# The second layer's router logits: product-and-sum on VectorE in place of transposes and matmuls on TensorE

## The reference, cut to what matters

```python
out[mask] = gate_w[mask, None] * (h @ w2[e])    # first layer: its output rows, y here
...
logits = x @ w_gate                             # second layer: x = y, (3072, 512) @ (512, 8)
flat = logits.flatten()
order = np.argsort(-flat)                       # greedy assignment by this order
```

## Time and profile before

| | |
|---|---|
| median of 3 runs | 1130.14 us (1125.43 to 1133.53) |
| the profiled execution's own time | 1124.73 us |
| its span | 1123.0 us |
| first layer's tiles | about 250 to 619 us of the span |
| TensorE busy, whole span | 933.2 us (83%) |
| VectorE busy, whole span | 592.6 us (53%) |
| mean granted clock of TensorE | 0.92 |

### The profile page before, as it was taken

How to read it: one execution, slowest core, us unless ns; L and a number is a source line. 1 busy time by engine, 2 the same in 40 slices (tenths; PEclk the granted TensorE clock), 3 DMA queues, 4 the chain that set the end, 5 groups by cost and what they waited for, 6 DMA issues and landing times.

```text
span 1123.0 us, 22070 instructions
## 1 busy us (share of the span) xinstructions
PE 933.2 (83%) x7642; PEld 767.9 (68%) x7643; DVE 592.6 (53%) x1728; ACT 320.9 (29%) x651; POOL 207.1 (18%) x291
## 2 busy tenths in 40 slices
PE   5998989617999999999997226797978889798995
PEld 4786878515888888888886215676666767576884
DVE  5767566575222222222221587777776777776550
ACT  3455454324222222222221021131313122224230
POOL 6644333001111111111110001020202020202021
PEclk9999999758999999999998556898999989899998
DMA  9668684604011111111110041414131221407110
GB/s 198 132 123 170 128 161 94 177 18 170 29 38 38 39 41 43 38 38 38 38 38 20 14 151 29 150 58 151 58 148 56 103 99 68 141 18 286 73 48 29
DMA packets 46015, 97.86 MB, mean 87 GB/s; under 512 B 7248, under 2 KB 19584, under 8 KB 45952
## 3 DMA queue, kind: packets, MB, share of 16 engines
q1 hardware_dynamic: 27200, 59.55, 18.4%
q0 software_dynamic: 8064, 26.46, 7.5%
q10 hardware_dynamic: 10688, 11.01, 4.8%
HBM read 77.49 MB, written 19.51 MB: 86 GB/s over the span
## 4 chain that ended last, share of the span: by engine, by line
PE 66%; DVE 23%; issue 4%; ACT 3%; DMA 2%; POOL 1%; DVEq 0%; ACTq 0%; SPq 0%; POOLq 0%
PE bank L760 25%; PE bank L899 9%; PE bank L914 9%; PE bank L672 3%; DVE w_low L1633 3%; PE bank L653 3%; PE bank L713 2%; PE bank L784 2%; PE bank L690 2%; DVE slot_hot L1613 2%; PE bank L807 2%; DVE ge L1503 2%; PE bank L662 2%; PE bank L922 1%; PE bank L850 1%
## 5 line engine op out<-in xcount | busy, mean ns | idle before, releaser
L899 PE MATMUL bank<-xh,w_high 128*128 128x384 f32 x256 | 94.7, 370 | 12.1 <-DVE xl L1637 7.2
L760 PE MATMUL bank<-w_high,hh 128*128 x200 | 83.2, 416 | 10.1 <-DVE hl L1397 10.1
L760 PE MATMUL bank<-w_high,xh 128*128 x200 | 82.5, 413 | 10.6 <-DVE gates L1390 10.6
L620 POOL DMA_INDIRECT out<-y_second,idx x24 | 25.2, 1048 | 354.8 <-ACT y_second L1041 352.4
L899 PE MATMUL bank<-xh,w_low 128*128 128x384 f32 x256 | 87.0, 340 | 0.0
L899 PE MATMUL bank<-xl,w_high 128*128 128x384 f32 x256 | 86.7, 339 | 0.0
L914 PE MATMUL bank<-w_high,hh 128*128 128x512 f32 x192 | 84.4, 439 | 0.0
L1041 ACT ACTIVATE w_high<-w_landed 128x1024 fp32r<-128x1024 f32 x64 | 63.9, 1049 | 59.7 <-DMA w_landed<-in_moe_w 59.7
L760 PE MATMUL bank<-w_high,hl 128*128 x200 | 80.7, 404 | 0.0
L760 PE MATMUL bank<-w_low,hh 128*128 x200 | 80.6, 403 | 0.0
L760 PE MATMUL bank<-w_low,xh 128*128 x200 | 80.0, 400 | 0.0
(11 more groups left out here) (290 smaller groups left out, 1960.4 us busy)
## 6 DMA issues: line engine op xcount, KB each, us to landing
w_landed<-in_moe_w SPq DMA_DIRECT2D x16, 2048.0 KB, 11.2
va<-in_v_win SPq DMA_DIRECT2D x16, 585.0 KB, 6.4
raw_w<-in_moe_w SPq DMA_DIRECT2D x4, 2048.0 KB, 12.2
k_raw<-in_k SPq DMA_DIRECT2D x16, 384.0 KB, 9.4
q_eye<-in_q ACTq DMA_DIRECT2D x16, 384.0 KB, 7.3
x_rows<-x ACTq DMA_DIRECT2D x12, 384.0 KB, 10.9
x_rows<-x SPq DMA_DIRECT2D x4, 387.0 KB, 8.0
xg<-x_rows,gidx POOLq DMA_INDIRECT x26, 3.4
```

Of the source, the lines that this page charges most:

```text
L620: pool.indirect_dma_start(out=out[:, :], out_offset=bass.IndirectOffsetOnAxis(ap=idx2[:, col:col + 1], axis=0), in_=y2[t][:, :], in_offset ...
L760: last = mm(ps, lhs[a][:, c, :], rhs[b](c), start=c == 0 and t == 0, stop=c == n - 1 and t == 2)
L899: last = mm(bank[fc % 2][:, 0:CAP], w[:, q % 2, c, f], a[:, c, :], start=c == 0 and t == 0, stop=c == KC - 1 and t == 2)
```

## The change

The second layer's logits of a tile are made on VectorE. For each of the eight router columns one `scalar_tensor_tensor` instruction multiplies the 128x512 tile of y with that column (the same in all partitions) and sums each row's products into one element of y's columns 512 to 519 (`accum_out`); the products themselves go to PSUM bank 6 or 7 in turn and are not read. The transposes of y (L800), their copy (`yt`) and the small matmuls (L807) go, and with them the pass of the pipeline that served the last tile. The eight instructions of tile i-1 stand at the end of VectorE's pass over tile i. The router is loaded as a 128x8x512 tile, each partition reading the same 16 KB; the load stands on SyncE's queue behind the two first weight loads and ahead of the last store of x. The host hands over the router transposed.

```diff
-        wg2 = sb("wg2", [P, KC, E])
...
-        yt = sf("yt", [P, KC, P])
+        wg2 = sf("wg2", [P, E, DM])
...
-        below = sb("below", [P, 68 * 256])
+        below = sb("below", [P, 68 * 256 + 16])
...
             for raw_, src in zip(raw, (w1, w2)):
                 sp.dma_start(raw_[:, :, :], src[0, :, :].rearrange("(c p) f -> p c f", p=P)).then_inc(guess_loaded, 16)
+            sp.dma_start(wg2[:, :, :], bass.AP(w_gate2.tensor, 0, [[0, P], [DM, E], [1, DM]])).then_inc(gate_loaded, 16)
             sp.wait_ge(x_ready, B)
             store_x(B - 1, HP - 1)
...
             def scatter(st, i):
-                pool.wait_ge(y_done[st] if st else l2_out, val(i + 1))
+                pool.wait_ge(l2_out, val(E * (i + 1)))
...
-            def transpose_y(i):
...
-            def second_logits(i):
-                pe.wait_ge(yt_out, val(i + 1))
-                pe.wait_ge(l2_out, val(i))
-                for c in range(KC):
-                    last = mm(bank[7][:, 0:E], yt[:, c, :], wg2[:, c, :], start=c == 0, stop=c == KC - 1)
-                last.then_inc(l2_done, 1)
...
-            def step1(i, cur=True, prev=True, prev2=True):
+            def step1(i, cur=True, prev=True):
                 if cur:
                     g, par = group_of(i)
                     up(0, i, g, par, 0)
-                if prev2:
-                    transpose_y(i - 2)
                 if prev:
                     transpose_h(0, i - 1)
                 if cur:
                     up(0, i, g, par, 1)
-                if prev2:
-                    second_logits(i - 2)
...
-            def step(st, i, cur=True, nxt=True, prev=True, prev2=True):
-                if prev2:
-                    act.wait_ge(yT_done, val(i - 1))
-                    act.wait_ge(l2_done, val(i - 2))
-                    copy(yt[:, :, :].rearrange("p c t -> p (c t)"), bank[6][:, :]).then_inc(yt_out, 1)
...
+            def second_logits(i):
+                dve.wait_ge(y_done[0], val(i + 1))
+                if not isinstance(i, int) or i > 0:
+                    dve.wait_ge(l2_out, val(E * i))
+                for e in range(E):
+                    if e >= 2:
+                        dve.wait_ge(l2_out, val(E * i + (e - 1)))
+                    stt(bank[6 + e % 2][:, :], y[:, 0:DM], 1.0, wg2[:, e, :], ALU.mult, ALU.mult, accum_out=y[:, DM + e:DM + e + 1]).then_inc(l2_out, 1)
+
+            def step(st, i, cur=True, nxt=True, prev=True):
                 if prev:
                     h_lo(st, i - 1)
-                if prev2:
-                    dve.wait_ge(l2_done, val(i - 1))
-                    vec.tensor_copy(y[:, DM:YW], bank[7][:, 0:E]).then_inc(l2_out, 1)
                 if cur and nxt:
                     x_lo(st, i + 1)
...
                     chain(vec.tensor_copy(gates[:, 0:1], gates[:, 1:2]))
                     chain(vec.tensor_copy(gates[:, 1:2], gates[:, 2:3]))
+                if prev:
+                    second_logits(i - 1)
...
+    laid["moe2_w_gate"] = _np.asarray(inputs["moe2_w_gate"]).T
```

More of the change, by code:

```diff
@@ L359, in two_layers_of_experts @@
         down_done, y_done = two("down_done"), two("y_done")
-        yT_done, yt_out, l2_done, l2_out = sem("yT_done"), sem("yt_out"), sem("l2_done"), sem("l2_out")
+        gate_loaded, l2_out = sem("gate_loaded"), sem("l2_out")
         l2_loaded = sem("l2_loaded")
@@ L413, in _ @@
             sp.dma_start(wg[:, :, :], w_gate.rearrange("(c p) e -> p c e", p=P)).then_inc(small_loaded, 16)
-            sp.dma_start(wg2[:, :, :], w_gate2.rearrange("(c p) e -> p c e", p=P)).then_inc(small_loaded, 16)
             sp.dma_start(bias2[:, :, :], bass.AP(modality_bias.tensor, 0, [[0, P], [E, 2], [1, E]])).then_inc(small_loaded, 16)
@@ L735, in unit @@
                 if n == 4:
-                    pe.wait_ge(small_loaded, 48)
+                    pe.wait_ge(small_loaded, 32)
                 if n >= 5:
@@ L794, in down @@
                 product(bank[5][:, :], (hh, hl), rhs, FC).then_inc(down_done[st], 1)
-            def transpose_y(i):
-                pe.wait_ge(y_done[0], val(i + 1))
-                pe.wait_ge(yt_out, val(i))
-                for c in range(KC):
-                    last = tr(bank[6][:, P * c:P * c + P], y[:, P * c:P * c + P], ident[:, :])
-                last.then_inc(yT_done, 1)
-            def second_logits(i):
-                pe.wait_ge(yt_out, val(i + 1))
-                pe.wait_ge(l2_out, val(i))
-                for c in range(KC):
-                    last = mm(bank[7][:, 0:E], yt[:, c, :], wg2[:, c, :], start=c == 0, stop=c == KC - 1)
-                last.then_inc(l2_done, 1)
             def group_of(i):
@@ L834, in _ @@
             pe.wait_ge(table_ready, 1)
-            step1(0, prev=False, prev2=False)
-            step1(1, prev2=False)
+            step1(0, prev=False)
+            step1(1)
             step1(2)
@@ L842, in _ @@
             step1(tiles, cur=False)
-            step1(tiles + 1, cur=False, prev=False)
             def count(ph, t):
@@ L1103, in split_next @@
                         split_hi(0, u, g + 1, np_)
-            step(0, 0, prev=False, prev2=False)
+            step(0, 0, prev=False)
             split_next(0)
-            step(0, 1, prev2=False)
+            step(0, 1)
             split_next(1)
@@ L1117, in _ @@
             step(0, tiles, cur=False)
-            step(0, tiles + 1, cur=False, prev=False)
             def hidden_high(q, fc):
@@ L1219, in token_biases @@
                 dve.wait_ge(const_ready, 2)
-                dve.wait_ge(small_loaded, 48)
+                dve.wait_ge(small_loaded, 32)
                 dve.wait_ge(modality_loaded, 16)
@@ L1444, in split_next @@
                         split_lo(0, u, g + 1, np_)
-            step(0, 0, prev=False, prev2=False)
+            step(0, 0, prev=False)
             split_next(0)
-            step(0, 1, prev2=False)
+            dve.wait_ge(gate_loaded, 16)
+            step(0, 1)
             split_next(1)
```

## The result

The changed kernel took 1173.39 us (median of four executions, 1169.40 to 1175.69), the kernel before 1129.42 in its four beside it (1125.43 to 1133.53): 1.0385 times as long, with a 95% interval of 1.0336 to 1.0434. It is slower, as forecast, by more than forecast: 1155 was predicted, in a range that reached to 1192. The profiled execution took 1169.4 us (span 1167.7).

What follows compares the result with a forecast made beforehand. VectorE's chain from y through eight products and `hl` to down was to replace TensorE as the bound: 16.6 (loop) + 5.2 (last interval) + 3.1 (tail) = +24.9 us on 1124.7, plus 5.4 to the median, 1155 us; range 1131 to 1192.

Steps and rivals of the forecast that it cites:

- TensorE's relief: First layer's loop: removed transposes and small matmuls save TensorE 1.49 us a pass, its need falling from 13.77 to 12.28.
- up to the first product: Loop period: from the start of y through the second copy of gates and a 0.05 hand-over, 1.25 us.
- the eight products to the end of the last sum: Loop period: eight VectorE instructions added between y and `hl`, 8t = 5.60 us.
- the turn: Loop period: VectorE's register load and two branches before `hl`, taken as 0.2 us, bounds 0 and 0.9.
- the hand-over: Loop period: from VectorE's `hl` to TensorE's down, estimated at 0.15 us; at half clock it had been 0.35.
- t = 0.70: VectorE's share per product instruction, in us, taken between bounds of 0.60 and 0.84.
- the upper bound of 0.84: Upper limit of t: an undivided instruction of 0.69 us followed by one of 0.15 for the sum.
- The rival of half pace: VectorE's products: two fp32 inputs with a sum run at half pace, t 1.14, +113 us, 1243; chance 0.04.
- The last interval and the tail: Loop's end: last y-to-y interval +5.2 us; from last y to the copy of the logits +3.1 us.
- At nothing: Terms put at no cost: y's scatter (1.6 us slack), the router's load, and the second layer's untouched rows.
- The clock: Rival: clock falls in TensorE's gap before down, 2.1 us per pass, +48, 1203, for t above 0.8; chance 0.08.
- The gap's length: First layer's loop: TensorE stands idle 2.2 us a pass in front of down.

Runs made afterwards that it cites:

- fill3: The changed kernel with TensorE's transposes of the next tile's inputs made four times over; 1161.52 us, 1.0251 of the kernel before.
- fill1: The changed kernel with TensorE's transposes of the next tile's inputs made twice over; 1155.63 us, 1.0228 of the kernel before.
- six: The changed kernel with six products per tile instead of eight, the last two experts' logits left out; 1123.13 us, 0.9952 of the kernel before.
- late_all: The changed kernel with all eight products made one pass later, ahead of the wait for down, and two y buffers; 1099.86 us, 0.9755 of before.
- one_y_two_places: The changed kernel with its last four products moved one pass later, single y buffer kept; 1127.56 us, 0.9998 of the kernel before.
- no_sum: The changed kernel without accum_out, the logits replaced by a copy of eight columns of y; 1155.38 us, 1.0224 of the kernel before.
- two_y: The changed kernel with two y buffers and a later scatter, no products moved; 1187.72 us, 1.0525 of the kernel before.
- two_places: The changed kernel with its last four products moved one pass later and two y buffers; 1102.19 us, 0.9775 of the kernel before.

## Why the prediction came out as it did

**What bounds, and what is added to it.** Right. The chain y, gates, eight products, `hl`, down became the bound, and TensorE's relief was lost in its gap. fill3 and fill1 (TensorE's work given back, same period), six (VectorE's work cut, shorter period) and late_all (same work, off the chain, 12.25 us) show it from three sides.

**The terms of the period**, predicted and measured: up to the first product 1.25 and 1.32; the eight products to the end of the last sum 5.60 and 5.30; the turn 0.2 and 0.31; `hl` 1.29 and 1.29; the hand-over 0.15 and 0.35; down 6.00 and 6.00. The sum was 14.49, the trace has 14.57. The products had been put too dear (t = 0.70 against 0.65), the turn and the hand-over too cheap, and the errors nearly cancel. The bound of 0.35 for the hand-over stood in the earlier trace rows; I had set it aside because it was at half clock, and it holds at full clock.

The Trainium skill (VectorE: DVE Perf Modes, "Two Vector instructions with no wait between them") calls such an instruction two, the main one and an accumulator read. The trace agrees, with its rows `DVE_READ_ACCUMULATOR` of 0.14 us; but they lie beside the next product, so the upper bound of 0.84, which put the two end to end, was not nearly reached.

The rival of half pace is refuted by the same rows: 0.644 us from start to start for 512 elements of two fp32 inputs with a sum, and 0.60 without. The Trainium skill (Vector Engine (DVE) Microarchitecture Reference, "7. Points that are easy to get wrong") says that two such sources in SBUF halve the throughput; here the measurement decides against it.

**The last interval and the tail**: +5.4 and +2.7 against +5.2 and +3.1. Right.

**At nothing**: the router's load and the scatter. Right; y waited for TensorE in every pass of the changed kernel's loop.

**The clock: the step that failed.** The prediction had the fall as a rival with a chance of 0.08, at 2.1 us each, which "comes into play for t above 0.8", since after a gap of 2.52 us matmuls ran at full clock. t was 0.65 and the gap 1.8 us, and the clock fell in nine passes of 23 all the same; the clock under 1.00 in the loop's windows, which the prediction had named as a sign that it was wrong, was there (0.95). One row after one gap had been taken for a limit. The changed kernel's own trace has the same gap of 2.52 us in front of the same instruction with a fall behind it, and the trace of before held a warning too: at the end of a gap of 2.30 us in the second layer the clock fell to half (a row of TensorE's timeline; then windows: us, PE busy, clock, DMA share, GB/s).

```profile
956.71 0.19 PE L880 MATMUL bank<-mineb,tri 128*128 128x24 bf16 x1 [2.30 <-DVE mineb L1592]
```

```profile
955.00:956.00 1.00, 0.00 (x0) 1.00 1.02 410
957.00:959.00 2.00, 0.00 (x0) 0.50 1.00 378
```

Over the kernels of this study the falls in the loop grow with the gap: none at 0.5 and at 1.37 us, none in 21 passes at 1.54 to 1.58, none in one at 1.67 (one_y_two_places), one in one at 1.84 (no_sum), nine in 22 at 1.79 to 1.86 (the change), fifteen in 22 at 2.37 us and more (two_y). The price of one was 1.54 us, less than the 2.1 from the earlier trace rows.

Without this step the sum would have held: of the 44.7 us between the profiled executions 13.9 are the nine falls and 5.2 the second layer, and the other 25.6 stand against a forecast of 24.9. That 1173 lies within the stated range is partly luck: the range left the clock's case out, and its upper part was meant for a dearer product.

**The gap's length.** Forecast at 2.2 us, it shows as 1.81, though 14.57 - 12.28 = 2.29 us should be left. The trace counts each matmul to its end, 0.39 us, where in a row the next one starts after 0.23, so an idle gap looks shorter than the time that it costs; that accounts for part of the difference.

**The second layer.** At nothing in the sum, and 5.2 us longer in the changed kernel's profiled execution, with none of its rows changed. Its time goes with the number of stretches at half clock between `smx` and the end, over all ten traces, the stretch that `smx` falls into counted too: seven in 496.3 us (before) and 497.7 (late_all), eight in 498.7 to 499.6 (one_y_two_places, six, no_sum), nine in 500.5 to 501.7 (the change, fill1, fill3, two_places, two_y). The two that the changed kernel has more are those behind the gap of 2.30 us that ends at 1057.43 and the one of 2.52 at 1099.38, whose counterparts before (1016.31 and 1056.54) had none. From the first of these points to the second it took 41.95 us against 40.23, and from there to the end 68.27 against 66.44, together 3.6 us of the 5.2; and the half-clock stretch at the layer's start ended 71.6 us after `smx` in place of 67.3, which goes with another 1.2.

**What stays open.** Why one gap brings a fall and an equal one not. In the changed kernel the falls come nearly in every other pass, in two_y in two or three passes running and then not in one, so it isn't chance from pass to pass, but no run was made to find what decides it. Nor does a run say why the second layer got its additional falls. Each kernel has one trace, and the executions of one kernel differ by some 8 us (before: 1125.43 to 1133.53), so a few us in one stage of one trace needn't be the edit's doing.

## What to carry to other kernels

Before giving an idle engine more work, find the cycle that the work enters. Here VectorE was idle for three quarters of the loop, and the place of eight instructions decided between 3.9% slower (between y and `hl`, on the way to TensorE) and 2.5% faster (ahead of a wait for TensorE). Taking work from TensorE pays only if it doesn't wait afterwards: a recurring gap costs its own length, and with some 1.8 us and more in this loop also stretches at half clock in some passes. A full-clock row behind one gap doesn't show that gaps of that length are safe: the same gap of 2.52 us was followed by full clock in one trace and by half clock in the other.

## What the runs showed of the hardware

- An instruction over 512 fp32 elements with both inputs in SBUF and the product to PSUM takes 0.60 us from start to start, 0.644 with `accum_out`; the accumulator's read, 0.14 us, starts together with the next instruction.
- The granted clock can fall from 2.4 to 1.2 GHz after a gap of 1.8 us in a loop of 14.6 us in which TensorE is otherwise busy, and it was back some 3.4 us later. The fall began up to 1.5 us after the matmuls had started again. At the same gap it fell in some passes and not in others, in a regular order. In the traces with gaps of 1.37 us, and of 1.54 to 1.58 us, it did not fall after one of them.
- The second layer's length followed the number of its half-clock stretches: 496.3 and 497.7 us with seven, 500.5 to 501.7 with nine.
- From the end of VectorE's `hl` to the start of the waiting matmul it was 0.35 us at full clock too.
- VectorE's sequencer needed 0.31 us for the turn of a hardware loop where nothing covers it (the change). In front of the first product it was 0.35 us with three register operations (two_y) and 0.13 with one (the change).
